# An xLSTM-style attention and two wide linear layers on one core: a new start for the first three units

## The reference

```python
for t in range(S):                                    # B=4, H=8, S=768, D=40
    m_new = maximum(f_gate[t] + m, i_gate[t])
    f_stab, i_stab = exp(f_gate[t] + m - m_new), exp(i_gate[t] - m_new)
    C = f_stab * C + i_stab * outer(v[t], k[t])       # D x D per batch and head
    n = f_stab * n + i_stab * k[t]
    h, nq = C @ q[t], n @ q[t]
    y[t] = sigmoid(o_gate[t]) * h / maximum(abs(nq), 1)
x = y as [B*S, H*D]                                    # 3072 x 320
x = maximum(0.01*(x @ w_in), x @ w_in) @ w_out         # d_ff = 2048
out = h2 * cos(h2) @ w2_out,  h2 = x @ w2_in           # d_ff = 2048
```

## Time and profile before

| | us |
|---|---|
| median of 3 runs | 844.53 (843.31 to 844.69) |
| the profiled execution's own time | 841.17 |
| its span, first to last instruction | 839.2 |
| PE busy | 815.4 |
| DVE, ACT, POOL busy | 646.0, 466.8, 321.1 |

### The profile page before, as it was taken

One profiled execution on the slowest core, in us unless ns is written; L12 is line 12 of the kernel. 1 busy time (PEld: TensorE's weight loads), 2 busy tenths in 40 slices (PEclk: granted clock), 3 DMA queues, 4 the chain that ended last, 5 costly groups with the idle time before them and its releaser, 6 DMA issues.

```text
span 839.2 us, 18203 instructions
## 1 busy us (share of the span) xinstructions
PE 815.4 (97%) x6908; PEld 782.5 (93%) x6908; DVE 646.0 (77%) x1394; ACT 466.8 (56%) x1050; POOL 321.1 (38%) x328
## 2 busy tenths in 40 slices
PE   7799899999999999999999999999999999999997
PEld 5788899999999999999999999999999999999997
DVE  5788777777787876777853488888888888888886
ACT  6255343433433434334336687777677767777776
POOL 5646434332222343322205643333333333333332
PEclk9799999999999999999999999999999999999999
DMA  8573822423444223235023320302020202010000
GB/s 276 167 204 95 214 78 79 125 78 87 140 121 129 85 79 125 79 85 187 2 77 107 105 108 1 119 1 72 1 71 1 71 1 71 2 66 6 16 9 24
DMA packets 37972, 70.58 MB, mean 84 GB/s; under 512 B 3584, under 2 KB 25088, under 8 KB 37888
## 3 DMA queue, kind: packets, MB, share of 16 engines
q1 hardware_dynamic: 37840, 69.40, 26.9%
q10 hardware_dynamic: 48, 0.05, 0.0%
HBM read 57.44 MB, written 11.99 MB: 83 GB/s over the span
## 4 chain that ended last, share of the span: by engine, by line
PE 85%; DVE 6%; issue 4%; ACT 4%; POOL 1%; POOLq 0%; DVEq 0%; ACTq 0%
PE h L593 30%; PE acc L605 12%; PE acc L607 11%; PE acc L606 11%; PE s L593 10%; PE s L535 2%; DVE kvo_s L991 2%; PE s L551 2%; PE s L563 2%; PE x L571 1%; DVE D L999 1%; ACT g_hi L728 1%; ACT kvo_s L728 1%; PE acc L675 1%; ACT kvo_s L735 1%
## 5 line engine op out<-in xcount | busy, mean ns | idle before, releaser
L593 PE MATMUL h<-xT,w_in 128*128 128x384 f32 x1536 | 306.7, 341 | 0.1
L593 PEld LDWEIGHTS h<-xT,w_in 128*128 128x128 f32 x1536 | 266.7, 188 | 3.3 <-DVE w_in L1176 0.4
L728 ACT ACTIVATE t_f<-h 128x384 f32<-128x384 f32 x192 | 94.4, 492 | 296.9 <-PE h L593 296.9
L605 PE MATMUL acc<-w_out,g_hi 128*128 128x320 f32 x768 | 241.6, 315 | 2.2 <-POOL g_lo L1407 1.8
L607 PE MATMUL acc<-w_out,g_lo 128*128 128x320 f32 x768 | 237.3, 309 | 0.0
L606 PE MATMUL acc<-w_out,g_hi 128*128 128x320 f32 x768 | 235.9, 307 | 0.0
L1407 POOL TENSOR_TENSOR g_lo<-g_f,g_hi 128x384 fp32r<-128x384 f32 x127 | 130.1, 1024 | 211.9 <-ACT g_hi L728 211.9
L1102 DVE TENSOR_TENSOR g_f<-h,t_f 128x384 f32<-128x384 f32 x128 | 71.2, 556 | 107.6 <-ACT t_f L728 107.5
L605 PEld LDWEIGHTS acc<-w_out,g_hi 128*128 128x128 f32 x768 | 144.2, 188 | 4.6 <-POOL g_lo L1407 2.0
L606 PEld LDWEIGHTS acc<-w_out,g_hi 128*128 128x128 f32 x768 | 144.4, 188 | 0.0
L607 PEld LDWEIGHTS acc<-w_out,g_lo 128*128 128x128 f32 x768 | 144.0, 188 | 0.0
(11 more groups left out here) (141 smaller groups left out, 785.7 us busy)
## 6 DMA issues: line engine op xcount, KB each, us to landing
qk_s<-qk SPq DMA_DIRECT2D x24, 512.0 KB, 3.9
kvo_s<-kvo SPq DMA_DIRECT2D x24, 484.0 KB, 6.2
x_dram<-stage SPq DMA_DIRECT2D x8, 960.0 KB, 6.2
xT<-x_dram SPq DMA_DIRECT2D x8, 960.0 KB, 4.9
D<-g_dram SPq DMA_DIRECT2D x42, 128.0 KB
qe<-q SPq DMA_DIRECT2D x24, 160.0 KB, 4.2
eG_b<-e_dram SPq DMA_DIRECT2D x48, 80.0 KB
out<-x SPq DMA_DIRECT2D x24, 160.0 KB, 1.8
```

What stands on the lines that cost most here:

```text
L593: last = nc.tensor.matmul(bank[:, 0:BLOCK], w(a), x[:, k, :], start=(n == 0), stop=(n == 7))
L605: nc.tensor.matmul(acc[t][:, 0:DM], g_hi[:, s, r], w_out[:, 0, j, :], start=(j == 0), stop=False)
L728: copy = lambda o, i, **k: nc.scalar.activation(o, i, ACT.Copy, **k)
```

## The change

- **Masks.** `hide` and a copy of the identity (`ident_r`) become fp32r, so that each `hide_later` is one matmul in fp32r instead of one in fp32.
- **Decays.** PE adds the keys' part of the decays into PSUM too (`spread_keys`: 8 recorded fp32 matmuls of 128x256, on all 128 rows, in two halves of 64 output partitions). DVE zeroes rows 32 to 127 of the operands by four memsets. `first_decays` is then one exponential of 128x512 per unit without a bias. `turn_columns(i_s, 0, 0)` isn't needed for it any more and moves, with its copy, from the head to slot 1; the two of the second half move from slot 0 to slot 1.
- **Scales.** For unit 0 PE spreads exp(G) (`spread_scales`, 8 recorded matmuls of 128x128) and ACT copies it to `eG_b`; for units 1 and 2 the store to HBM and the loads are issued by ACT instead of SP.
- **Order.** i - m goes from DVE to POOL, unit 0's keys from POOL to DVE; the sigmoid's reciprocal is cut into halves in every unit, of which the second runs after the probs (in the slots: at the end of the PROBS slot). In units 0 and 1 POOL multiplies the gate by the normaliser (`gated`) in place of DVE's division of the outputs. All engines' lists for the units 0 to 2 are reordered, with other `WARM` counts.
- **Weights.** `LATE_IN`, `LATE_OUT`, SP's list of loads and POOL's list of splits change. The semaphore of a unit's inputs is split by tensor.

The diff, cut:

```diff
-LATE_IN = {2: 2, 3: 3, 5: 4, 7: 5, 9: 6, 11: 7}
-LATE_OUT = {4: 2, 6: 3, 8: 4, 10: 5, 12: 6, 14: 7}
+LATE_IN = {1: 2, 2: 3, 5: 4, 6: 5, 9: 6, 10: 7}
+LATE_OUT = {3: 2, 6: 3, 7: 4, 10: 5, 11: 6, 14: 7}
-WARM = (2, 3, 3, 5, 5)
+WARM = (5, 4, 6, 8, 3)
-        hide = sb("hide", [P, SUB])
+        hide = sb("hide", [P, SUB], F32R)
+        pairs = x1[:, 1, 0:GROUPS * PACK * HD].rearrange("p (g n) -> p g n", g=GROUPS)
+        ident_r = g_hi[:, 0, 0:P]
+        i_all = stage_f[:, 2, :]
+        keep_all = r_f[:, 0, :]
...
# SP
-            load_unit_inputs(0, 0)
+            load_qk(0, 0)
             sp.dma_start(f_s[:, half_cols(1)], ...)
             sp.dma_start(i_s[:, half_cols(1)], ...)
+            load_kvo(0, 0)
+            load_q3(0, 0)
             load_unit_inputs(0, 1)
-            sp.wait_ge(gate_exp, 1)
-            store_gates(e_dram, keep[:, 0:TILES, :], 0).then_inc(e_stored, 16)
             load_unit_inputs(0, 2)
-            sp.wait_ge(e_stored, 16)
-            load_unit_scales(0, 0)
-            load_unit_scales(0, 1)
-            load_unit_scales(0, 2)
             load_raw_in(w1i, 0)
+            load_raw_out(w1o, 0)
+            sp.wait_ge(G_done, 1)
             store_gates(g_dram, ..., 0).then_inc(g_stored, 16)
             load_raw_in(w1i, 1)
-            load_raw_out(w1o, 0)
             load_raw_out(w1o, 1)
...
             load_unit_decays(0, 3)
             load_raw_in(w1i, 2)
+            load_unit(0, 4)
             load_raw_in(w1i, 3)
-            load_unit(0, 4)
             load_raw_out(w1o, 2)
+            load_raw_out(w1o, 3)
             load_raw_in(w1i, 4)
-            load_raw_out(w1o, 3)
             load_raw_in(w1i, 5)
             load_unit(0, 5)
             load_raw_out(w1o, 4)
             load_raw_in(w1i, 6)
+            load_raw_in(w1i, 7)
             load_raw_out(w1o, 5)
-            load_raw_in(w1i, 7)
...
# PE
+            def spread_keys(c):
+                for u in range(SUBS):
+                    t = (c * SUBS + u) * SUB
+                    for e in range(2):
+                        queries = acc[c][side(e), :].rearrange("p (h u t) -> p u h t", h=SIDE, u=SUBS)[:, u]
+                        last = nc.tensor.matmul(queries, i_all[:, t:t + SUB], sel[:, :, side(e)], start=False, ...)
+                last.then_inc(bc_done, 1)
+            def spread_scales():
+                for g in range(GROUPS):
+                    last = nc.tensor.matmul(h_bank[0][0:ROWS, g * CHUNK:(g + 1) * CHUNK], pairs[:, g, :], keep_all[:, 0:CHUNK], ...)
+                last.then_inc(eG_spread, 1)
             spread_decays(0)
             pe.wait_ge(i_step, 2)
-            turn_columns(i_s, 0, 0)
+            pe.wait_ge(blank_done, 4)
+            spread_keys(0)
             unit_scores(0, 0)
             pe.wait_ge(gate_exp, 2)
-            pe.wait_ge(cols_done, 1)
             turn_columns(f_s, 1, 0)
+            pe.wait_ge(pairs_done, 1)
+            spread_scales()
+            unit_state(0, 0)
             spread_decays(1)
-            spread_decays(2)
+            spread_keys(1)
             unit_scores(0, 1)
-            unit_state(0, 0)
-            unit_scores(0, 2)
-            unit_state(0, 1)
-            pe.wait_ge(cols_done, 2)
-            pe.wait_ge(dx_done, 2 * TILES)
             unit_carried(0, 0)
             unit_within(0, 0)
+            unit_state(0, 1)
+            spread_decays(2)
+            spread_keys(2)
+            unit_scores(0, 2)
             unit_state(0, 2)
-            warm_up(WARM[1], acc[2])
             unit_carried(0, 1)
             unit_within(0, 1)
+            pe.wait_ge(dx_done, TILES)
+            warm_up(WARM[1], acc[2])
...
# PE, slot 1 instead of slot 0
                     pe.wait_ge(gate_exp, 4)
-                    pe.wait_ge(x1_done, TILES)
+                    pe.wait_ge(xT_done, TILES)
+                    turn_columns(i_s, 0, 0)
                     turn_columns(i_s, 0, 1)
                     turn_columns(f_s, 1, 1)
...
# ACT
+            def first_decays(c):
+                act.wait_ge(bc_done, c + 1)
+                nc.scalar.activation(D[:, c, :, :]..., acc[c][:, :], ACT.Exp).then_inc(dx_done, 1)
             gate_scale(0)
+            store_scales()
+            gate_weights(0)
+            first_decays(0)
             sigmoid_exp(0, 0)
-            gate_weights(0)
-            column_copy(0, 0)
-            first_decays(0, 0)
-            first_decays(0, 1)
             column_copy(1, 0)
+            first_scales()
+            first_state()
+            load_scales(1)
+            load_scales(2)
+            first_decays(1)
...
# DVE, slots: half 0 after SCORES, half 1 after PROBS
                 if u := row.unit(i, SCORES):
-                    sigmoid(*u)
+                    sigmoid(*u, 0)
+                if u := row.unit(i, PROBS):
+                    sigmoid(*u, 1)
...
# DVE, first units
             gate_maxima(1)
-            sigmoid(0, 0)
             first_probs(0)
-            gate_decays(1)
+            first_keys()
+            sigmoid(0, 0, 0)
             state(0, 0)
+            sigmoid(0, 0, 1)
             first_probs(1)
+            sigmoid(0, 1, 0)
             state(0, 1)
-            first_probs(2)
             normaliser(0, 0)
-            sigmoid(0, 1)
-            outputs(0, 0)
+            first_probs(2)
+            sigmoid(0, 1, 1)
             state(0, 2)
+            outputs(0, 0)
+            gate_decays(1)
             normaliser(0, 1)
-            x_lo(0, 0, xT[:, 0])
+            sigmoid(0, 2, 0)
             outputs(0, 1)
-            sigmoid(0, 2)
+            sigmoid(0, 2, 1)
+            x_lo(0, 0, xT[:, 0])
             normaliser(0, 2)
+            normalised(0, 2)
             x_lo(0, 1, xT[:, 0])
             outputs(0, 2)
             x_lo(0, 2, xT[:, 0])
...
# POOL
+            def gated(b, c):
+                pool.wait_ge(nrm_done, unit(b, c) + 1)
+                pool.wait_ge(sig_done, 2 * unit(b, c) + 2)
+                nc.gpsimd.tensor_tensor(o, o, nrm...to_broadcast([P, HEADS, HD]), ALU.mult).then_inc(gated_done, 1)
-            second_rates()
             first_columns(0)
-            first_keys(0)
+            first_keys(1)
             first_scaled(0)
-            first_keys(1)
             own_state(0, 0)
+            first_keys(2)
             first_scaled(1)
             own_state(0, 1)
-            first_keys(2)
+            gated(0, 0)
+            second_rates()
             first_scaled(2)
             own_state(0, 2)
+            gated(0, 1)
             split_in_lo(0)
             second_inputs()
...
+            unit_weights(0, 4)
             split_out_lo(3)
-            unit_weights(0, 4)
             split_out_lo(4)
             unit_masks(0, 4)
+            unit_weights(0, 5)
             split_out_lo(5)
-            unit_weights(0, 5)
```

More of the change, by code:

```diff
@@ L509, in unit_scores @@
                 p = c % BUFS
-                pe.wait_ge(unit_in[p], unit_loaded(b, c))
+                pe.wait_ge(qk_in[p], unit_loaded(b, c))
+                if first(b, c) and c == 1:
+                    pe.wait_ge(eG_done, 1)
                 if first(b, c) and c == 2:
-                    pe.wait_ge(dx_done, 4)
+                    pe.wait_ge(dx_done, 2)
                 if not first(b, c):
@@ L613, in turn_columns @@
                 for c in range(TILES * SUBS):
[L614 removed]
+                    at, t = columns_at(k, half) + c * n, (half * TILES * SUBS + c) * SUB
                     for e in range(2):
@@ L649, in slot @@
                     block_transpose(row.block(i) - 1, t)
-                if row.starts(0, i) and i == 0:
+                if row.starts(0, i) and i == 1:
                     pe.wait_ge(gate_exp, 4)
-                    pe.wait_ge(x1_done, TILES)
+                    pe.wait_ge(xT_done, TILES)
+                    turn_columns(i_s, 0, 0)
                     turn_columns(i_s, 0, 1)
@@ L873, in slot @@
                         copy(x2[:, t, 0:DM], acc[t][:, 0:DM]).then_inc(acc_read, 1)
-                if row.starts(0, i) and i == 0:
+                if row.starts(0, i) and i == 1:
+                    column_copy(0, 0)
                     column_copy(0, 1)
@@ L985, in _, with sigmoid @@
             first_columns()
-            def sigmoid(b, c):
-                o = o_s[:, c % BUFS, :]
-                u = unit(b, c)
-                dve.wait_ge(eo_done, u + 1)
+            def sigmoid(b, c, half):
+                o = o_s[:, c % BUFS, half * (DM // 2):(half + 1) * (DM // 2)]
+                dve.wait_ge(eo_done, unit(b, c) + 1)
                 nc.vector.reciprocal(o, o).then_inc(sig_done, 1)
@@ L1334, in unit_weights @@
                 mask(c)
-                keys(c)
-                carried(c)
+                keys(b, c)
+                carried(b, c)
             def unit_masks(b, c):
```

208 lines of the change are left out of this document (131 added, 77 removed).

## The result

The changed kernel takes **847.25 us** in the median of 8 runs (845.68 to 849.73), the kernel before 843.57 (841.08 to 844.69, 8 runs on the same chip): ratio 1.0046, 95% interval 1.0032 to 1.006. It is slower by 0.5%, where 833.5 us and "faster" were forecast.

What follows compares the result with a forecast made beforehand. PE was taken as the bound from the first slot on; -2.7 - 0.8 + 0.8 - 0.2 - 1.25 - 2.6 - 4.3 = -11.05 us, so 844.53 becomes 833.5 us, range 830 to 838.5.

Steps and rivals of the forecast that it cites:

- Masks, G, spreads: Head's start: masks end by 6.2 us, G at 7.0, unit 0's state product starts at 11.3 instead of 15.86.
- The 0.4 us allowed for a slow start: Head: added for the clock still at the lower level in part of the first spreads, ends 0 and 2 us.
- The end of the head: From unit 2's probs at 21.4 us DVE's list bounds; first product at 35.5 us instead of 38.23, -2.7 us.
- From there PE has ... 7.3 us: Head: PE's own work from unit 0's state product through unit 2's scores, ending at 19.4 us.
- The first product at full clock, and columns: First product at full clock, -0.8 us; 72 column matmuls instead of 48 in slot 1, +0.8 us.
- Block 0, -1.25 and -2.6: Holes before block 0's state products close: -1.25 us for unit 3, -2.6 us with 0.5 given back for units 4 and 5.
- issue plus 4.5 us ... up to 6.5 us: Unit 3, block 0: raw_in 3, issued at about 39.5 us, lands at 44 us, later as the ring is full.
- rival 1: ACT and the weights become the new wait: raw_in 3 and 5 land 2 us later, +3, 836.5 us; 13%.
- Rival 5: Moving the split has no effect as POOL's mask is late; half of block 0's holes go, +2, 835.5 us; 5%.
- Later blocks, -4.3: 12 holes of 0.37 us at PE's state product go, -4.4, with 0.1 back for 20 more DVE instructions.
- The cover named: Later blocks: after the change the state ends some 0.4 us before PE's carried states (L551) need it.
- Rival 2: Holes move: the second half reciprocal delays the state, PE waits at L551; later blocks' 4.3 us stay, 837.8 us; 12%.

Runs made afterwards that it cites:

- e9: e6 with one table changed (LATE_IN 1, 2, 4, 6, 8, 12, so piece 3 is split in slot 2, piece 4 in slot 4); 838.66 us, ratio 0.9947.
- e4: The changed kernel with the second half reciprocal between `g_f` and `g_lo` of the slot after the probs; 840.23 us, ratio 0.9967.
- e3: The changed kernel, first four weight pieces held until unit 1's exponential is made, unit 2's exponential ahead of ACT's first split; 844.41 us, ratio 1.0025.
- e6: The changed kernel with e3's and e4's edits, piece 3 loaded before unit 4, `w_out`'s piece 5 before `w_in`'s 7, other split slots; 834.87 us, ratio 0.9895.
- e10: The changed kernel with e3's hold of weight pieces, e4's place of the half reciprocal, and weight slots and lists of before; 834.12 us, ratio 0.9896.
- e7: The kernel before with only the reciprocal halved, the second half between `g_f` and `g_lo` of the outputs slot; 838.83 us, ratio 0.9945.
- e8: The kernel before with only the reciprocal halved, the second half at the end of the probs slot; 847.23 us, ratio 1.0047.
- e11: The kernel before with only the reciprocal halved, the second half behind `g_lo` instead of ahead of it as in e7; 840.04 us, ratio 0.9964.
- e12: The kernel before with the whole reciprocal moved to where e7 has the second half; 842.02 us, ratio 0.9993.
- e1: The changed kernel with the slots' reciprocal whole again, in the scores slot; 846.78 us, ratio 1.0038.
- e2: The changed kernel with `w_in`'s weight piece 3 loaded before unit 4's inputs; 846.16 us, ratio 1.0038.
- e5: The changed kernel with the weight slots, SP's list of loads and POOL's list of splits as before; 845.29 us, ratio 1.0019.

## Why the prediction was wrong

**Masks, G, spreads: right in this execution, and partly by luck.** Masks ended at 5.7 us (forecast 6.2). G came at 6.9 (7.0): `stage` of L1024 took 1.24 us beside POOL's i - m, 0.69 over its 0.55, where 0.8 was taken. The keys' eight matmuls took 1.08 us (0.95), so pairs on different halves do run together. An exponential took 0.60 us (0.63), unit 0's state product started at 11.69 us (11.3). But of the nine profiled executions with this head only two (the changed kernel and e9) reached it then; the other seven did at 13.15 to 15.33 us, because the spread and the key sums took up to twice as long. In e4:

```profile
7.06 2.05 PE L706 MATMUL acc<-t_f,x 128*128 128x128 f32 x8 [1.29 <-DVE t_f L1029]
9.04 1.98 PE L715 MATMUL acc<-x,stage 128*64 128x256 f32 x8
```

The 0.4 us allowed for a slow start was too small for those. The granted clock reads 1.00 from 7 to 11 us in all nine executions, and also from 4 to 10 us in the kernel before, where the masks took 0.91 us per 512 columns and the prediction took PE to be at the lower level. So the granted clock does not show this slowness, and which of PE's two levels it was stays open.

**The end of the head: wrong, -2.7 came out as +1.4.** "From there PE has ... 7.3 us" left out that unit 1 needs its scales from HBM. ACT's DMA issues were charged with their issue time alone, not with their landing behind the 1.4 MB of weights that SP now issues ahead of them. With that removed e3, e6 and e10 start the first product at 36.3 to 36.4 us, within a microsecond of the forecast 35.5; e9, the one among them whose unit 0 came at 11.69 us, has unit 2's state product at 21.36 us (forecast 21.4) and the first product at 34.99. The second step that failed follows from the first: the end of the head was counted as DVE's, but from 24 to 36 us PE was busy all 12.00 us at the lower level, its `warm_up` matmuls between 27 and 39 us alone 8.0 us. The count of DVE's list, "11.75 us", was of the right size: from unit 2's state product to the first product e3 takes 13.75 us, where 21.4 to 35.5, 14.1 us, was forecast. The head's length also differs between executions of unchanged code: 38.2, 40.2, 41.7, 41.9 and 40.6 us in before, e7, e8, e11 and e12. The reference profile was a favourable one, which the prediction could have asked about, since it lay 3.4 us below the median. Against the median of these five, 40.6 us, the changed head (39.7 us, the median of after, e1, e2, e4 and e5) gains some 0.9 us, a third of the forecast; the +1.4 is one profile against one.

**The first product at full clock, and columns: right.** 16 matmuls took 3.05 us, where 8 had taken 2.79; 72 column matmuls took 2.27 us against 1.57 for 48, +0.7 where +0.8 was taken. The lower level had moved to 24 to 36 us, though, behind the wait of 3.11 us.

**Block 0, -1.25 and -2.6: wrong.** For unit 3 "issue plus 4.5 us ... up to 6.5 us" was mis-sized: piece 3 was issued at 43.46 us, 4 us later than counted, and landed 8.21 us after that. Of the 4 us, 3.8 are SP's list starting at 36.14 instead of 32.38 us, behind the second store of exp(G): the prediction took the old time of issue over, though the change moves that store. ACT waited 4.26 us, PE 3.47 us, and the clock then fell, so that unit 3's carried states came at 61.37 us instead of 57.36. That is rival 1, whose +3 us was still too small: it counted no fall of the clock. Unit 4's hole did go, unit 5's shrank to 1.0 us, but the waits at the transposition grew from one of 1.0 us to three, 1.9 us in all, and 0.4 us for `Cm` came. Rival 5 is not borne out: with the split moved unit 4 has no hole in the changed kernel, e2, e3, e4 and e6.

**Later blocks, -4.3 came out as +0.8: a step that alone turned the sign (e4).** The holes were measured rightly, 12 of 0.37 us: without them e4, e6, e7, e9, e10 and e11 take 312.3 to 312.5 us instead of 316.7, which is 4.3 us. The cover named was rightly chosen as well, since PE never waits at the carried states there. What was not followed is what else starts from the state: POOL's `Cm`, decay sum, mask, keys and `qe`, and through them DVE's second `g_lo` and the outputs, which reached PE 0.06 us before it turned them. The rows of before would have shown this; "what is late next" was asked of L551 alone. Rival 2 had the mechanism, a later state, and the price, but the wrong place.

**The forecast's sum** would have been -11.05 us; e10, with the second half behind the state and the weights held, stands 8.1 us under the before of its own runs (842.19). What is missing is mostly block 0, 66.4 us in e10's profile where the forecast would have 61.6.

**Open.** Why e1 needs 317.4 us from unit 6 to 23 where the kernel before, with the same reciprocal, needs 316.7: its holes are 0.36 instead of 0.30 us. Why the profile shows PE at two speeds in the first 12 us while the granted clock stays at 1.00. And which of the earlier DMAs holds up the store of exp(G).

**Why units 4 and 5 still wait 1.5 us in e7 and e10.** Both have the old lists, so half the reciprocal and the whole split still lie before the probs. In e7 at unit 4:

```profile
66.20 0.63 ACT L776 ACTIVATE D<-D 128x512 f32<-128x512 f32 x1 [0.92 <-POOL D L1253]
66.74 0.83 ACT L728 ACTIVATE w_in<-raw_in 128x768 fp32r<-128x768 f32 x1
67.60 1.32 DVE L1183 TENSOR_TENSOR w_in<-raw_in,w_in 128x768 fp32r<-128x768 f32 x1 [0.77 <-ACT w_in L728]
```

ACT waits 0.92 us for POOL's mask before exp(D), its rounding of the weight piece comes behind that, and DVE's split waits 0.77 us for the rounding. So the 1 us that the half reciprocal freed becomes a wait, and the probs start at 68.95 us, as before (68.94).

## What to carry to other kernels

Before an operation is moved, list everything that starts from what stands behind it, on all engines, and read the slack of each from the trace: the first wait that disappears is not the bound, the smallest slack behind it is. A load costs its landing behind what is in flight ahead of it, here on another engine's queue too, and not only the time of its issue; the median landing in a quiet stretch is no estimate for a full one. The moment of its issue moves with whatever the list ahead of it waits for. Where DVE must wait for POOL's product anyway, an operation with one SBUF input can run in that time.

## What the runs showed that was not expected

- A small transfer issued by ACT was not spared by being on another queue than SP's weight pieces: a load of 80 KB took 6.03 us with them in flight, and at most 3.3 us without them.
- A weight piece of 384 KB landed 8.2 to 9.5 us after its issue in block 0, where 4.5 us was the median in the head and block 0 of before; seven DMAs of a unit and several pieces were ahead of it.
- The granted clock fell to the lower level after PE had waited 3.11 us in a head full of small matmuls, and stayed there for 12 us although PE was busy in all of them. After a wait of 0.93 us at the same place (e3) it stayed at 0.94 for the stretch. A long wait is not needed, though: in the kernel before it fell between 20.0 and 20.5 us, after a wait of 1.62 us that ended at 18.99.
- The same eight recorded matmuls of the spread took 1.13 us in two executions of the new head and 2.05 us in seven, with the granted clock at 1.00 from 7 to 11 us in all nine.
